# Range reduction of cos(h) in turns of 2 pi: the whole turns on VectorE, their subtraction on GpSimd, absolute value and sine at one place on ScalarE

## What is computed

```python
# q, k, v: (4, 8, 576, 64)
scores = scale * q @ k.T
kth = np.partition(scores, -32, axis=-1)[..., -32:-31]
scores = np.where(scores >= kth, scores, -1e9)
attn = softmax(scores);  x = attn @ v            # 2304 tokens x 512
h = x @ w_in                                     # 512 -> 2048
x = (h * np.cos(h)) @ w_out                      # 2048 -> 512
e = argmax(x @ w_gate)                           # 8 experts
out = prob[e] * sigmoid(x @ w_output_gate)[e] * (relu(x @ w1[e]) @ w2[e])
```

## Time and profile before

| | us |
|---|---|
| median of 3 runs (lowest, highest) | 1443.74 (1442.76, 1446.47) |
| the profiled execution | 1439.62 |
| its span, first to last instruction | 1438.0 |
| TensorE matmuls busy | 1275.0 |
| VectorE busy | 933.8 |
| ScalarE busy | 655.6 |
| GpSimd busy | 560.5 |

### The profile page before, as it was taken

How to read it: one execution, slowest core, us unless ns; L and a number is a source line. 1 busy time by engine, 2 the same in 40 slices (tenths; PEclk the granted TensorE clock), 3 DMA queues, 4 the chain that set the end, 5 groups by cost and what they waited for, 6 DMA issues and landing times. The chain is left out here.

```text
span 1438.0 us, 18220 instructions
## 1 busy us (share of the span) xinstructions
PE 1275.0 (89%) x5962; PEld 805.4 (56%) x5963; DVE 933.8 (65%) x1690; ACT 655.6 (46%) x1082; POOL 560.5 (39%) x696
## 2 busy tenths in 40 slices
PE   4557899999999999899899998899599999999996
PEld 2435656857647658567567576584244444444443
DVE  6999998899999999999899999533111111111110
ACT  3455665766666766766757666542011111111110
POOL 2444562464554654554554645515211111111110
PEclk9768999999999999999999999999799999999998
DMA  8201001101001100100010000003313433251000
GB/s 247 88 8 24 1 8 36 37 8 39 9 16 33 32 16 8 25 23 18 17 47 1 1 15 1 8 8 132 136 59 119 149 141 141 80 181 49 14 13 1
DMA packets 81839, 71.52 MB, mean 50 GB/s; under 512 B 62266, under 2 KB 62266, under 8 KB 81248
## 3 DMA queue, kind: packets, MB, share of 16 engines
q1 hardware_dynamic: 76192, 60.86, 13.2%
q0 software_dynamic: 5568, 9.65, 2.1%
HBM read 62.97 MB, written 11.45 MB: 52 GB/s over the span
## 5 line engine op out<-in xcount | busy, mean ns | idle before, releaser
L720 DVE MAX8 tops<-scores_left 128x8 f32<-128x576 f32 x432 | 327.2, 758 | 12.3
L407 POOL TENSOR_TENSOR probs<-scores,probs 128x576 f32<-128x576 f32 x144 | 212.3, 1474 | 241.5 <-ACT probs L514 241.5
L976 PE MATMUL dense_banks<-x_T,weights 128*128 128x256 f32 x1024 | 249.4, 399 | 17.0 <-ACT h_T L552 17.0
L864 DVE COPY x_gathered_T<-score_banks 128x512 f32<-128x512 f32 x25 | 17.3, 691 | 347.6 <-PE score_banks L1100 347.6
L986 PE MATMUL dense_banks<-weights,h_T 128*128 128x512 f32 x512 | 236.4, 605 | 0.0
L976 PEld LDWEIGHTS dense_banks<-x_T,weights 128*128 128x128 f32 x1024 | 198.4, 199 | 59.6 <-ACT h_T L552 21.1
L723 DVE MATCH_REPLACE8 scores_left<-tops,scores_left 128x576 f32<-128x576 f32 x288 | 213.8, 742 | 0.0
L1126 PE MATMUL dense_banks<-weights,expert_h_T 128*128 x400 | 178.2, 598 | 17.4 <-DVE expert_h_T L869 17.3
L1110 PE MATMUL score_banks<-weights,x_gathered_T 128*128 x400 | 178.5, 600 | 1.1 <-DVE x_gathered_T L864 1.1
L514 ACT ACTIVATE probs<-scores,top_consts 128x576 f32<-128x576 f32 x144 | 111.5, 775 | 122.3 <-POOL top_consts L404 122.0
L986 PEld LDWEIGHTS dense_banks<-weights,h_T 128*128 128x128 f32 x512 | 93.5, 193 | 107.0 <-issue 107.0
(11 more groups left out here) (160 smaller groups left out, 1544.9 us busy)
## 6 DMA issues: line engine op xcount, KB each, us to landing
weights<-in_moe_w SPq DMA_DIRECT2D x16, 2048.0 KB, 10.9
y_rows<-y_rows_sb SPq DMA_DIRECT2D x18, 256.0 KB, 2.0
k_rows<-in_k SPq DMA_DIRECT2D x32, 128.0 KB, 2.7
q_rows<-in_q SPq DMA_DIRECT2D x16, 256.0 KB, 3.5
v_rows<-in_v SPq DMA_DIRECT2D x32, 128.0 KB, 2.4
weights<-in_moe_w_in SPq DMA_DIRECT2D x1, 4096.0 KB, 13.0
weights<-in_moe_w_out SPq DMA_DIRECT2D x1, 4096.0 KB, 22.5
k_rows<-in_k SPq DMA_DIRECT2D x16, 32.0 KB, 2.6
```

What stands on the lines that cost most here:

```text
L407: nc.gpsimd.tensor_tensor(ex, SS[:, u % 3, i, :], ex, ALU.subtract).then_inc(s["masked_done"], 1)
L720: V.max(top, src).then_inc(s["tops_done"], 1)
L976: last = MM(HO[:, f % 2, 0:BT], win[:, kd, f * P:(f + 1) * P], XT[:, m % 2, kd, :], start=kd == 0, stop=kd == KD - 1)
```

## The change

h is kept in whole turns. `copy_h` multiplies by 1/(2 pi) while it copies (an activation in place of a copy), and `copy_y` multiplies by 2 pi again, since the gated h carries the factor through the product. VectorE's `whole_turns` adds and takes off 1.5 x 2^23 in one instruction with floating output, which leaves the nearest whole number. The subtraction is GpSimd's new `fold`, four pieces of 128x512, in the same step (i = 2, 4): two ahead of the scaling of the probabilities and two behind it. The sine scales by 2 pi. On ScalarE, absolute value and sine of both halves of a piece stand together between `copy_scores` and `exps` of the next step (i = 3, 5). GpSimd's second gate piece moves ahead of the denominators.

```diff
 def gate(st, piece):
-    pool.wait_ge(s["cos_done"], m * 8 + 4 * g + 2 + piece // 2 + 1)
+    pool.wait_ge(s["cos_done"], m * 8 + 4 * g + piece // 2 * 2 + 2)
+def fold(st, piece):                        # GpSimd
+    for m, i in block_at(st):
+        if i in (2, 4):
+            g = (i - 2) // 2
+            if piece == 0:
+                pool.wait_ge(s["turns_done"], 2 * m + g + 1)
+            f = g * 8 + piece * 2
+            r = R[:, g, piece * 2:piece * 2 + 2, :]
+            nc.gpsimd.tensor_tensor(r, HS[:, f:f + 2, :], r, ALU.subtract).then_inc(s["reduced_done"], 1)
 # GpSimd, step st
                 gate(st, 0)
+                gate(st, 1)
...
-                gate(st, 1)
...
                 gate(st, 2)
+                fold(st, 0)
+                fold(st, 1)
...
                 gate(st, 3)
+                fold(st, 2)
+                fold(st, 3)
 # ScalarE
-    copy(HS[:, f, :], HO[:, f % 2, 0:BT])
+    nc.scalar.activation(HS[:, f, :], HO[:, f % 2, 0:BT], ACT.Copy, scale=1.0 / TWO_PI)
-    nc.scalar.activation(r, r, ACT.Sin, bias=half_pi[:, 0:1], scale=-1.0)
+    nc.scalar.activation(r, r, ACT.Sin, bias=half_pi[:, 0:1], scale=-TWO_PI)
 # ScalarE, step st, between copy_scores(st) and exps(st - 2, 1)
                     if i in (3, 5):
-                        sine(m, (i - 3) // 2, 1)
+                        for h in range(2):
+                            absolute(m, (i - 3) // 2, h)
+                            sine(m, (i - 3) // 2, h)
...
-                    if i in (2, 4):
-                        absolute(m, (i - 2) // 2)
...
-                    if i in (2, 4):
-                        sine(m, (i - 2) // 2, 0)
 # VectorE
-    V.tensor_scalar(r1.bitcast(I32), hs, 1.0 / TWO_PI, None, ALU.mult)
-    V.scalar_tensor_tensor(out=r1, in0=r1.bitcast(I32), scalar=-TWO_PI, in1=hs, op0=ALU.mult, op1=ALU.add)
+    V.tensor_scalar(r1, hs, ROUND, -ROUND, ALU.add, ALU.add)
```

More of the change, by code:

```diff
@@ L57 @@
 BIG = 2.0 ** 80
+ROUND = 1.5 * 2.0 ** 23
 BLOCK = 2
@@ L551, in copy_h @@
                 act.wait_ge(s["dense_filled"], m * MOE_FILLS + f + 1)
-                copy(HS[:, f, :], HO[:, f % 2, 0:BT]).then_inc(s["dense_emptied"], 1)
+                nc.scalar.activation(HS[:, f, :], HO[:, f % 2, 0:BT], ACT.Copy, scale=1.0 / TWO_PI).then_inc(s["dense_emptied"], 1)
             def copy_y(t):
@@ L558, in copy_y @@
                     act.wait_ge(s["small_filled"], SMALL["t", t - 2] + 1)
-                copy(YN[:, t % 2, :], HO[:, t % BLOCK, :]).then_inc(s["dense_emptied"], 1)
+                nc.scalar.activation(YN[:, t % 2, :], HO[:, t % BLOCK, :], ACT.Copy, scale=TWO_PI).then_inc(s["dense_emptied"], 1)
             def copy_keys(b, p):
@@ L574, in copy_logits, with absolute @@
                 copy(L[:, t, :], small(("g", t))[:, 0:2 * E]).then_inc(s["small_emptied"], 1)
-            def absolute(m, g):
-                act.wait_ge(s["reduced_done"], m * 4 + 2 * g + 2)
-                for h in range(2):
-                    r = R[:, g, h * 4:h * 4 + 4, :]
-                    nc.scalar.activation(r, r, ACT.Abs).then_inc(s["cos_done"], 1)
+            def absolute(m, g, h):
+                act.wait_ge(s["reduced_done"], m * 8 + 4 * g + 2 * h + 2)
+                r = R[:, g, h * 4:h * 4 + 4, :]
+                nc.scalar.activation(r, r, ACT.Abs).then_inc(s["cos_done"], 1)
             def sine(m, g, h):
-                act.wait_ge(s["cos_done"], m * 8 + 4 * g + h + 1)
+                act.wait_ge(s["cos_done"], m * 8 + 4 * g + 2 * h + 1)
                 r = R[:, g, h * 4:h * 4 + 4, :]
-                nc.scalar.activation(r, r, ACT.Sin, bias=half_pi[:, 0:1], scale=-1.0).then_inc(s["cos_done"], 1)
+                nc.scalar.activation(r, r, ACT.Sin, bias=half_pi[:, 0:1], scale=-TWO_PI).then_inc(s["cos_done"], 1)
             def late_copy(t, quarter):
@@ L655, in _ @@
                     copy_keys(b, p)
-                for m, i in dense:
-                    if i in (2, 4):
-                        sine(m, (i - 2) // 2, 0)
                 if st >= LOOP - 2:
@@ L736, in reduce_h @@
                 r1 = R[:, g, :, :].rearrange("p a n -> p (a n)")
-                V.tensor_scalar(r1.bitcast(I32), hs, 1.0 / TWO_PI, None, ALU.mult).then_inc(s["reduced_done"], 1)
-                dve.wait_ge(s["reduced_done"], m * 4 + 2 * g + 1)
-                V.scalar_tensor_tensor(out=r1, in0=r1.bitcast(I32), scalar=-TWO_PI, in1=hs,
-                                       op0=ALU.mult, op1=ALU.add).then_inc(s["reduced_done"], 1)
+                V.tensor_scalar(r1, hs, ROUND, -ROUND, ALU.add, ALU.add).then_inc(s["turns_done"], 1)
             for st in range(LOOP):
@@ L746, in _ @@
                     if i in (2, 4):
-                        reduce_h(m, (i - 2) // 2)
+                        whole_turns(m, (i - 2) // 2)
                 if 0 <= st - 1 < NS:
@@ L765, in late_reduce @@
                 r = R16[:, g * 8:(g + 1) * 8, :]
-                V.tensor_scalar(r.bitcast(I32), hs, 1.0 / TWO_PI, None, ALU.mult).then_inc(s["reduced_done"], 1)
+                V.tensor_scalar(r, hs, ROUND, -ROUND, ALU.add, ALU.add).then_inc(s["reduced_done"], 1)
                 dve.wait_ge(s["reduced_done"], n + 1)
-                V.scalar_tensor_tensor(out=r, in0=r.bitcast(I32), scalar=-TWO_PI, in1=hs,
-                                       op0=ALU.mult, op1=ALU.add).then_inc(s["reduced_done"], 1)
+                V.tensor_tensor(r, hs, r, ALU.subtract).then_inc(s["reduced_done"], 1)
             def choose(ts):
```

15 lines of the change are left out of this document (8 added, 7 removed).

## The result

The changed kernel takes 1505.37 us (median of 4 runs, 1503.60 to 1505.74); the kernel before took 1443.25 beside it (4 runs, 1440.78 to 1446.47). The ratio is 1.0427, 95% interval 1.0404 to 1.0449: **62 us slower**. The profiled execution took 1505.74 us.

The account below looks back on a forecast made before the run. VectorE was taken to set the pace, with the denominators' loop 2 us behind. Eight blocks losing 6.3 us (50) plus 3 us of carry gave +54, 1498 us against the median of 1443.7; range 1470 to 1520.

Parts of the forecast that it names:

- the denominators' loop: VectorE's scores, masks, exponentials, denominators, back to VectorE's reciprocals: claimed as second bound, 2 us behind VectorE.
- a saving per reducing step: VectorE drops its scalar_tensor_tensor, 2.20 us per half block, 16 times: 35 us, at the worst 18.
- The walk through m=4: Steps 45 to 48 of one clean dense block, followed before and after: the block loses 6.3 us.
- first wait: VectorE's wait at the reciprocals in step 46, after the block's first reduction: claimed 4.0 us.
- second: VectorE's wait at the reciprocals in step 48, after the block's second reduction: claimed 6.7 us.
- ScalarE's lump: Two Abs, one load and one Sin more between copy of scores and exponential: 4.53 us more on the loop.
- the folds ahead of top_consts: GpSimd's four subtractions per half block, 5.1 us, all queued ahead of the next top_consts, for which ScalarE waits.
- the carry from block to block: TensorE and ScalarE enter the next block up to 4 us behind VectorE: 7 x 0.45 = 3 us.
- the less clean block: Block m=5, where the slack is gone: VectorE already waited 1.92 us at the reciprocals before the change.
- the loop is not waited for: Rival: VectorE keeps its 2.20 us per reduction, 35 us faster, 1409 us; chance 9%.
- the first wait doesn't carry over: Rival: GpSimd and ScalarE recover before step 48, both halves lose 1.8 us, 29 in all, 1473 us; chance 13%.
- Table load: ScalarE's loads on the loop: summed without drain; with 1.38 us drain each, 22 us beyond the sum.

Follow-up runs that it names:

- run 12: The changed kernel measured once more, unaltered: 1498.51 us, against 1439.52 for the kernel before beside it.
- Run 9: The kernel before with VectorE's scalar_tensor_tensor in the loop left out, output not the reference's: 1417.89 us against 1439.56.
- run 1: The kernel before with both absolute values and both sines moved to the head of the next step, no folds: 1487.54 us against 1446.23.
- run 5: The changed kernel with GpSimd's folds in the loop left out, output not the reference's: 1466.13 us against 1445.34 for the kernel before.
- run 7: The changed kernel with Exp in place of Sin, so no table loads in the loop: 1456.16 us against 1445.34 for the kernel before.
- Run 8: The changed kernel with absolute value, load and sine cut into 1024-column pieces at the tails of four steps: 1530.20 us against 1445.34 for the kernel before.
- run 3: The changed kernel with absolute values and sines moved behind the exponential and two copies of h: 1489.40 us against 1446.23 for the kernel before.
- Runs 1 to 8: Eight follow-up variants of the kernel before or the changed kernel, altering place of absolute values and sines, folds or table loads: 1453.06 to 1530.20 us.
- runs 9 to 12: Two kernels before without VectorE's second operation, one rearranged changed kernel, and the changed kernel repeated: 1417.89, 1416.46, 1444.87 and 1498.51 us.

## Why the prediction was right, and where it was not

It said 1498 us (1470 to 1520) and slower; 1505.37 was measured, 1498.51 in run 12. The mechanism held, and two of its sizes were too small and offset each other: waits and saving.

- **The bound.** VectorE paces the loop, and the denominators' loop lies 2 us behind it: right, in the clean blocks. Run 9 shows it from the other side: with the saving alone the waits grow from 12.5 to 29.5 us.
- **Prices.** Tensor_scalar with two additions 1.26 us (taken as 1.23), fold 1.27 (1.27), a saving per reducing step of 2.33 (2.20). Over the loop the saving is 43 us, not 35, because of the six longer instructions of before, which the prediction's clean block does not show. For the copies of h with a factor, 374 ns in place of 361 (1.7 us in all 128), I had put nothing.
- **The walk through m=4.** `Below` 3.55 us behind VectorE's step (3.26), first wait 4.44 (4.0), second 6.77 (6.7), hidden products after a pause of 6.79 (6) at 5.48 us and a clock of 0.67 (6.12, 0.60), block 6.5 us longer (6.3). Between copy of scores and exponential stand six instructions, as its own sum has them, not the seven that it names. Its terms stand one by one: ScalarE's lump (run 1), the folds ahead of top_consts (run 5), the loads in full (run 7). The second `below` comes 5.9 us behind VectorE's step (639.82, 633.93), as it did in the walk (608.2, 602.29).
- **The term that was mis-sized** is the carry from block to block, 7 x 0.45 = 3 us in the sum. Counted from one first reduction to the next, the blocks m=0 to 6 are 7.6, 8.4, 7.2, 8.3, 6.5, 9.6 and 7.3 us longer, 54.8 together, 7.8 in the mean, not 6.3 and 6.75: m=4, on which I walked, is the cheapest of all. What I had put down as a carry is, as I read it, for the most part a later head of ScalarE in the blocks where the next batch's keys are transposed. The timeline of ScalarE in step 37, block m=3, whose VectorE step starts at 483.08:

```profile
488.64 0.59 ACT L580 COPY k_T<-small_banks 128x512 f32<-128x512 f32 x1 [0.31 <-PE small_banks L908]
489.28 0.79 ACT L531 ACTIVATE probs<-scores,top_consts 128x576 f32<-128x576 f32 x1
```

  `Below` starts 6.2 us behind the step there, in m=4 2.4 (594.98, step 592.59). Such a head was late before the change too, by 5.0 us (464.86, step 459.83) where m=4 had 0.3 (561.34, step 561.07), so these blocks had less slack to begin with. Mask and folds end later by the same, and the first waits of m=1, 3, 5 and 6 are 7.0 to 8.3 us where I had 4.0. I had seen the less clean block and used it as evidence for a rival, not in the sum. The bill: waits of 114.5 us in all where I forecast 80 to 90. The sum still came near, since in such blocks part of the wait stands in place of something that was there before: a wait (2.3 us in m=1, 0.9 and 1.9 in m=5) or one of the six longer instructions, which all lie in m=1, 3, 5 and 6. That these offset each other was luck.
- **Behind the loop.** Up to the first hidden products of the late tiles (989.4, before 930.0) the kernel is 59.4 us longer, of the span's 66.2; the other 6.8 are no work of the change but a stretch in which ScalarE stands, told of below. That run 12, which lacks it, took the forecast's 1498 to within 1 us is luck: the kernel before took 1439.52 beside it, 4 us less than the forecast started from, and up to those hidden products run 12 is 61.9 us longer, not 54.
- **The rivals.** That the loop is not waited for fell with the first row of waits. That the first wait doesn't carry over: the second waits are 6.8 to 7.6 us in all blocks, it does. TensorE is not the bound: it works 92.70 of 105.86 us in the block.
- **Table load.** The rows put 612.88 - 611.59 = 1.29 us between the start of a load and the next instruction, as before. The drain of some 1.38 us that the Trainium skill (ScalarE: Activation LUTs, "What ACT_TABLE_LOAD costs") adds is not there. By the Trainium skill's total of 2.66 us for a load with its drain, as an estimate, run 7 would have gained 16 x 2 x 2.66 = 85 us; it gained 49, and the measurement decides.
- **The lock.** Top_consts in the reducing step still stands under VectorE's tensor_scalar, 1.08 us at 598.53, and the mask behind it is 1.41 long where it was 2.66 (in step 47 a mask still takes 2.14). The Trainium skill (SBUF — State Buffer, "Who interferes with whom") says that VectorE holds the port that it shares with GpSimd in an instruction with two SBUF inputs or in a two-port mode, and both rows fit that.

```profile
598.53 1.08 POOL L406 TENSOR_TENSOR top_consts<-tops,top_factors 128x2 f32<-128x2 f32 x1
600.85 1.41 POOL L409 TENSOR_TENSOR probs<-scores,probs 128x576 f32<-128x576 f32 x1 [1.24 <-ACT probs L531]
```

**What stays open.** No version was found that keeps VectorE's saving and has r in time for ScalarE's pauses; that there is none is not shown. What each fold costs in the blocks that lag was not measured block by block. That a mask of GpSimd under way makes VectorE's reducing instructions longer is read from their coincidence; no run took the mask away.

## What to carry to other kernels

Before work is moved between engines to unload the one that paces, measure how far behind it the next loop lies: for each value that the pacing engine takes, the time it was fetched less the time it was ready. Here that was 2 us in steps of 11.5; 4.5 us more in it, and 3 us of another engine's work ahead of its head, cost 62 us though the pacing engine had 43 less to do. Look for a place where the engine waits already: that is where the absolute values stood before. Run 8 shows that cutting a lump up can be worse, and run 3 that moving it along can move the wait along. And walk through the worst block as well as the clean one.

## What was not expected of the hardware

In the changed kernel's profile ScalarE stands for 5.83 us behind the loop, at a copy of logits that no engine of the profile releases; in run 12, the same kernel, it does not. The two rows:

```profile
1065.10 0.17 ACT L592 COPY logits<-small_banks 128x16 f32<-128x16 f32 x1 [5.83 <-remote]
```

```profile
1061.87 0.17 ACT L592 COPY logits<-small_banks 128x16 f32<-128x16 f32 x1 [0.20 <-PE small_banks L1022]
```

Runs 1 to 8 have a gap there too, whatever the kernel, at this copy or the one behind it, with TensorE standing for 4.3 to 7.2 us. From the first hidden products of the late tiles to the end, their profiles take 513.4 to 515.4 us and the changed kernel's 514.8, those of runs 9 to 12 and of the kernel before 507.8 to 508.0. The medians of the kernel before were 1445 to 1446 us beside runs 1 to 8 and 1439.5 beside runs 9 to 12. So the gap goes with the chip or the time of the run and should drop out of those ratios. For the main comparison this is less sure: the changed kernel's profile has the gap, that of the kernel before has not, and the median before, 1443.25, lies between. Without it the change still costs 59 us (run 12). Its cause stays open.

The tensor_scalar with two float additions takes 1.23 us for 2048 columns in 15 of 16 cases (1.82 in one, hence the mean of 1.26), the same as the one with a single multiplication. TensorE's granted clock was 0.67 of its 2.4 GHz in the 5.48 us behind a pause of 6.79. Before, it was 0.60 in the 6.11 behind two pauses of 2.3 us with 1.2 of work between them. The one longer pause did not cost more.
